# An RWKV scan with two MLPs behind it: operands fetched by another queue, scores loaded in halves, and three steps put in another order

## The reference

```python
for t in range(S):
    y[:, :, t] = np.einsum('bhd,bhde->bhe', rt, state)
    Sa = np.einsum('bhde,bhe->bhd', state, at)
    state_decay = state * wt[:, :, None, :] - np.einsum('bhd,bhe->bhde', Sa, bt)
    state = state_decay + np.einsum('bhd,bhe->bhde', vt, kt)
...
h = x @ w_in                              # 3072 x 320 by 320 x 2048
x = np.maximum(0.01 * h, h) @ w_out       # by 2048 x 320
gate = 1.0 / (1.0 + np.exp(-(x @ w_gate)))
out = (gate * (x @ w_val)) @ w_out2       # 320 x 1536, 1536 x 320
```

## Time and profile before

| | us |
|---|---|
| median of the runs | 1144.23 (1143.53 to 1144.45) |
| profiled execution | 1153.02 |
| its span | 1151.3 |
| PE busy | 1068.9 (93%) |
| DVE busy | 588.7 (51%) |
| ACT busy | 397.3 (35%) |
| POOL busy | 107.2 (9%) |

### The profile page before, as it was taken

How to read it: one execution, slowest core, us unless ns; L and a number is a source line. 1 busy time by engine, 2 the same in 40 slices (tenths; PEclk the granted TensorE clock), 3 DMA queues, 4 the chain that set the end, 5 groups by cost and what they waited for, 6 DMA issues and landing times.

```text
span 1151.3 us, 36471 instructions
## 1 busy us (share of the span) xinstructions
PE 1068.9 (93%) x16102; PEld 913.3 (79%) x16102; DVE 588.7 (51%) x1306; ACT 397.3 (35%) x782; POOL 107.2 (9%) x99
## 2 busy tenths in 40 slices
PE   2477889999999999999999999999999999999998
PEld 1477778888888877777888787888888888888887
DVE  6697957667675765656756123443223232323222
ACT  2232433434444533443342335542223222222222
POOL 6022020202021110101000000000000000000000
PEclk9989879999999999999999999999999999999999
DMA  5648263345436352635243123330100102020000
GB/s 180 207 128 217 60 176 81 115 104 153 122 94 173 91 138 57 166 79 143 43 125 80 42 91 119 106 88 1 60 1 5 55 1 60 1 60 1 23 1 23
DMA packets 134987, 99.82 MB, mean 87 GB/s; under 512 B 96560, under 2 KB 111920, under 8 KB 134832
## 3 DMA queue, kind: packets, MB, share of 16 engines
q1 hardware_dynamic: 132384, 85.06, 27.7%
q0 software_dynamic: 2448, 12.45, 3.1%
HBM read 78.61 MB, written 18.87 MB: 85 GB/s over the span
## 4 chain that ended last, share of the span: by engine, by line
PE 80%; issue 8%; DVE 6%; DMA 2%; POOL 2%; ACT 1%; SPq 1%; ACTq 0%; DVEq 0%; POOLq 0%
PE bank L736 16%; PE bank L787 11%; PE pair L787 11%; PE bank L751 4%; PE bank L807 4%; PE bank L805 4%; PE bank L806 4%; PE bank L752 4%; PE bank L753 4%; DVE prod L1173 2%; DVE t_unit L1177 2%; PE bank L712 2%; PE bank L755 2%; PE bank L756 2%; PE bank L559 2%
## 5 line engine op out<-in xcount | busy, mean ns | idle before, releaser
L1222 DVE TENSOR_TENSOR g_lo<-g_full,g_hi 128x512 fp32r<-128x512 f32 x168 | 120.9, 720 | 243.5 <-ACT g_hi L992 243.4
L992 ACT CAST g_hi<-g_full 128x512 fp32r<-128x512 f32 x168 | 104.4, 621 | 134.7 <-DVE g_full L1274 131.6
L736 PE MATMUL bank<-x_hi,w_up 128*128 128x512 f32 x480 | 136.2, 414 | 2.1 <-issue 2.1
L985 ACT ACTIVATE g_full<-bank 128x512 f32<-128x512 f32 x96 | 57.5, 598 | 215.6 <-PE bank L736 208.7
L1173 DVE TENSOR_TENSOR prod<-t_unit,p_unit 128x126 f32<-128x126 f32 (+22 forms) x372 | 103.6, 278 | 37.3 <-DMA p_unit<-p_dram 26.1
L1177 DVE TENSOR_TENSOR t_unit<-t_unit,prod 128x126 f32<-128x126 f32 (+22 forms) x372 | 105.3, 283 | 12.8
L736 PEld LDWEIGHTS bank<-x_hi,w_up 128*128 128x128 f32 x480 | 86.0, 190 | 21.5 <-issue 2.5
L736 PE MATMUL bank<-x_lo,w_up 128*128 128x512 f32 x288 | 83.7, 400 | 0.0
L1274 DVE TENSOR_TENSOR g_full<-pair,h_sb 128x512 f32<-128x512 f32 x36 | 24.9, 691 | 112.8 <-PE pair L787 112.0
L751 PE MATMUL bank<-g_hi,w_dn 128*128 128x512 f32 x192 | 77.4, 403 | 2.0 <-DVE g_lo L1222 1.8
L752 PE MATMUL bank<-g_hi,w_dn 128*128 128x512 f32 x192 | 75.6, 394 | 0.0
(11 more groups left out here) (143 smaller groups left out, 2357.4 us busy)
## 6 DMA issues: line engine op xcount, KB each, us to landing
b_sb<-in_bF SPq DMA_DIRECT2D x12, 512.0 KB, 6.0
a_sb<-in_aF SPq DMA_DIRECT2D x24, 256.0 KB, 6.4
k_sb<-in_kF SPq DMA_DIRECT2D x12, 512.0 KB, 4.8
p_unit<-p_dram SPq DMA_DIRECT2D x24, 256.0 KB, 4.2
v_sb<-in_vF SPq DMA_DIRECT2D x12, 512.0 KB, 6.7
r_sb<-in_rF SPq DMA_DIRECT2D x12, 512.0 KB, 8.1
w_raw<-in_wF SPq DMA_DIRECT2D x20, 260.0 KB, 3.4
stage<-in_w_out POOLq DMA_DIRECT2D x7, 640.0 KB, 4.5
```

What stands on the lines that cost most here:

```text
L736: last = nc.tensor.matmul(up_bank(m)[:], lhs, rhs, start=(e == 0), stop=(e == len(products) - 1))
L992: nc.scalar.copy(g_hi[:, m % 2], g_full[:]).then_inc(g_hi_ready, 1)
L1222: nc.vector.tensor_tensor(g_lo[:, m % 2], g_full[:], g_hi[:, m % 2].bitcast(F32), ALU.subtract).then_inc(g_lo_ready, 1)
```

## The change

The loads of k, b and a, apart from the first ones, are issued by GpSimd, each just after the wait for the product that frees the buffer (`fetch_k`, `fetch_b`, `fetch_a`, with semaphores of their own); SP keeps the first loads. The scores are read back in two halves of 16 rows, the upper half as soon as they are stored and the columns that used the old upper half are done; the lower half when the inverse before has ended. `inverse_first` waits for the upper half, and column 16 for the lower. `act_t_unit` moves from slot 6 to slot 7, behind the copies of kb. In slot 6 of VectorE `dve_y` comes ahead of `dve_decay`. The first `act_x` moves behind `act_u` of window 2. On SP's queue `store_y(n + 1)` is ahead of `load_w(n + 7)`. Three numbers of `FILL` fall.

```diff
@@ gpsimd_program
+                n = 2 * g
+                if g >= 0:
+                    fetch_k(pool, g + 1)
+                    fetch_b(pool, g + 2)
+                if g == 0:
+                    fetch_a(pool, 4)
+                if unit_in(g + 1):
+                    pool_k(pool, n + 2)
+                if unit_in(g + 2):
+                    pool_b(pool, n + 4)
+                    pool_a(pool, n + 4)
+                if g >= 0:
+                    fetch_a(pool, n + 5)
...
+                if g >= 0:
+                    fetch_a(pool, n + 6)
...
+        def fetch_k(pool, u):
             if unit_in(u):
 
-                multiplied(sp, "kb", 2 * (u - 1) + 1)
-                sp.dma_start(k_sb[:].rearrange("p c q t -> p (c q t)"),
-                             kF[u].rearrange("p c q t -> p (c q t)")).then_inc(k_loaded, 16)
+                multiplied(pool, "kb", 2 * (u - 1) + 1)
+                nc.gpsimd.dma_start(k_sb[:].rearrange("p c q t -> p (c q t)"),
+                                    kF[u].rearrange("p c q t -> p (c q t)")).then_inc(k_fetched, 16)
...
+        def load_p_rows(sp, rows, signal):
+            for z in range(2):
+                sp.dma_start(p_unit[z * MX:(z + 1) * MX, rows].rearrange("p s t -> p (s t)"),
+                             p_dram[:, rows].rearrange("m s t -> m (s t)")).then_inc(signal, 16)
+
+        def load_p_top(sp, u):
             if unit_in(u):
                 sp.wait_ge(p_stored, 128 * (u + 1))
 
+                if u > 0:
+                    sp.wait_ge(column_ready, (C - 1) * (u - 1) + C // 2)
+                load_p_rows(sp, slice(0, C // 2), p_top_loaded)
+
+        def load_p_low(sp, u):
+            if unit_in(u):
+
                 wait(sp, column_ready, (C - 1) * u)
...
@@ FILL
-                ("first", 0): 2, ("cross", 0): 14, ("ut", 0): 4, ("vrur", 0): 6,
+                ("first", 0): 2, ("cross", 0): 2, ("ut", 0): 4, ("vrur", 0): 6,
...
-                ("first", 2): 2, ("cross", 2): 14, ("ut", 2): 4, ("vrur", 2): 4,
+                ("first", 2): 2, ("cross", 2): 4, ("ut", 2): 4, ("vrur", 2): 4,
...
-                ("first", 4): 2, ("cross", 4): 24}
+                ("first", 4): 2, ("cross", 4): 4}
@@ scalar_program
-                    if s == 1 and g % 2 == 0 and 1 <= g // 2 <= NJ:
+                    if s == 1 and g % 2 == 0 and 2 <= g // 2 <= NJ:
                         act_x(act, g // 2 - 1)
...
                             act_u(act, n)
+                            if g == 2:
+                                act_x(act, 0)
                             act_ut(act, n)
...
-                    elif s == 6 and later:
-                        act_t_unit(act, g + 2)
-                    elif s == 7 and soon:
-                        act_kb(act, n + 2)
-                        act_kb(act, n + 3)
+                    elif s == 7:
+                        if soon:
+                            act_kb(act, n + 2)
+                            act_kb(act, n + 3)
+                        if later:
+                            act_t_unit(act, g + 2)
@@ inverse_first, inverse_columns
-            dve.wait_ge(p_loaded, 32 * (u + 1))
+            dve.wait_ge(p_top_loaded, 32 * (u + 1))
...
+                if t == C // 2:
+                    dve.wait_ge(p_low_loaded, 32 * (u + 1))
@@ vector_program, slot 6
-                    elif s == 6 and unit_in(g + 3) and n + 6 >= 4:
-                        dve_decay(dve, n + 6)
...
+                    elif s == 6:
+                        if now:
+                            dve_y(dve, n + 1)
+                        if unit_in(g + 3) and n + 6 >= 4:
+                            dve_decay(dve, n + 6)
```

More of the change, by code:

```diff
@@ L138, in rwkv_mlp_kernel @@
         k_loaded = sem("k_loaded")
+        a_fetched = [sem(f"a_fetched{i}") for i in range(4)]
+        b_fetched = [sem(f"b_fetched{i}") for i in range(2)]
+        k_fetched = sem("k_fetched")
         r_loaded = sem("r_loaded")
@@ L149, in rwkv_mlp_kernel @@
         p_stored = sem("p_stored")
-        p_loaded = sem("p_loaded")
+        p_top_loaded = sem("p_top_loaded")
+        p_low_loaded = sem("p_low_loaded")
         zeros_set = sem("zeros_set")
@@ L286, in pool_a @@
             u, c = divmod(n, 2)
-            pool.wait_ge(a_loaded[n % 4], 16 * (u // 2 + 1))
+            if n < 4:
+                pool.wait_ge(a_loaded[n], 16)
+            else:
+                pool.wait_ge(a_fetched[n % 4], 16 * (n // 4))
             pool.wait_ge(decay_ready, n + 1)
@@ L293, in pool_b @@
             u, c = divmod(n, 2)
-            pool.wait_ge(b_loaded[u % 2], 16 * (u // 2 + 1))
+            if u < 2:
+                pool.wait_ge(b_loaded[u], 16)
+            else:
+                pool.wait_ge(b_fetched[u % 2], 16 * (u // 2))
             pool.wait_ge(inv_ready, n + 1)
@@ L300, in pool_k @@
             u, c = divmod(n, 2)
-            pool.wait_ge(k_loaded, 16 * (u + 1))
+            if u == 0:
+                pool.wait_ge(k_loaded, 16)
+            else:
+                pool.wait_ge(k_fetched, 16 * u)
             pool.wait_ge(inv_ready, n + 1)
@@ L332, in gpsimd_program @@
             for g in range(-2, NU):
[L333 to L338, removed]
+                n = 2 * g
[11 more added lines that the diff above has]
+                    fetch_a(pool, n + 5)
+                if unit_in(g + 1):
+                    pool_k(pool, n + 3)
+                if unit_in(g + 2):
+                    pool_b(pool, n + 5)
+                    pool_a(pool, n + 5)
+                if g >= 0:
+                    fetch_a(pool, n + 6)
                 if g == -1:
-                    pool.wait_ge(p_loaded, 32)
+                    pool.wait_ge(p_low_loaded, 32)
                     for i in range(4):
@@ L408, in store_p @@
                 if c == 0:
-                    wait(sp, p_loaded, 32 * u)
+                    wait(sp, p_top_loaded, 32 * u)
+                    wait(sp, p_low_loaded, 32 * u)
                 dst = p_dram.rearrange("(h i c q) s t -> h i c s q t", h=2, i=2, c=2)
@@ L490, in sync_program @@
             load_a(sp, 1)
-            load_k(sp, 0)
+            load_k(sp)
             load_w(sp, 2)
@@ L498, in sync_program @@
             store_p(sp, 1)
-            load_p(sp, 0)
+            load_p_top(sp, 0)
+            load_p_low(sp, 0)
             load_v_tok(sp, 0)
@@ L1315, in vector_program @@
                         dve_vrur(dve, n + 1)
-                    elif s == 6 and now:
-                        dve_y(dve, n + 1)
+                    elif s == 6:
[3 more added lines that the diff above has]
+                            dve_decay(dve, n + 6)
                     elif s == 7 and later:
```

42 lines of the change are left out of this document (22 added, 20 removed).

## The result

The changed kernel takes 1179.2 us (median of 4 runs, 1176.11 to 1183.31) against 1144.1 us (1143.53 to 1144.45) of the kernel before on the same chip: a ratio of 1.031, 95% interval 1.028 to 1.034, slower by 35 us. The profiled execution took 1179.12 us, its span 1177.1 us.

What follows compares the result with a forecast made beforehand. From 210 us on TensorE's stream of MLP products bounds the kernel; before, engines wait in a ring. Start -16, boundaries +35, clock +15, less 2 absorbed, on the 1144.2 us median gave 1176 us, range 1141 to 1190.

Steps and rivals of the forecast that it cites:

- The start, -16: First three windows, before the MLP has work: first MLP product 16 us earlier, bounds -10 and -21.
- TensorE follows: Window 0: TensorE keeps up with columns starting 7 us earlier, since k is fetched some 7 us earlier.
- the halves of the scores cost nothing at the boundaries: Eight later boundaries: t_unit's store comes some 3 us later, but the zeroing needing it is 9 us later too.
- near 152: Sign of being right: the first MLP product near 152 us.
- its sign of being wrong at this step: Start: first MLP product after 158 us, with GpSimd waiting for k or VectorE for `p_unit`.
- x would bind in window 2: Window 2: x, landing at 158.15, is the next bound; first MLP product at 161.6 instead of 167.66, 6.1 us.
- The link between fills and fetches: Window 0: k is fetched earlier, and the 12 fills removed were 12 of 14 filling TensorE's wait for a, ka.
- The boundaries, +35: Eight boundaries, windows 2 to 9: late zeroing and collisions make TensorE wait for `g_lo`, seven of 4.8 us, one 3.1.
- The four collisions: Each boundary: GpSimd's multiplies k, b, a, k fall on VectorE's columns, 0.92 us each, 3.7 us together.
- rival 3: GpSimd's fetches land 4.3 us later in the first three windows, taking 13 of the 16 back: 1189 us; 8 in 100.
- The clock, +15: Behind the eight boundary waits: clock falls of 2.5 us each, 20, less 5 already there; bounds 0 and +21.
- rival 1: Boundaries: multiplies miss the columns, each costs only the later zeroing's 1.3 us, no clock fall: 1138 us; 17 in 100.

Runs made afterwards that it cites:

- Experiment 8: Experiment 3 with SP's reload of T ahead of the load of the lower half of the scores; 0.997 of the kernel before.
- 10 to 12: Experiment 3 with v, r, v_nu held until k landed and T's reload before the lower half: 0.991; plus decay ahead of y: 0.995; or first x split early: 0.992.
- experiment 12: Experiment 3 with v, r, v_nu held until k landed, T's reload before the lower half, and first x split ahead of the u copies again; 0.992 of the kernel before.
- experiment 3: Changed kernel with t_unit zeroed behind the kb copies only up to g = 1, in slot 6 from window 2 on; 1.000 of the kernel before.
- experiment 4: Changed kernel with GpSimd's multiplies held until column 13 of the inverse from window 2 on, zeroing still late; 1.009 of the kernel before.
- experiment 2: Kernel before with one part of the change alone, the zeroing of t_unit behind the kb copies; 1.039 of the kernel before.
- experiment 9: Kernel before with only the 42 fewer fills of the cross products; 0.997 of the kernel before.
- experiment 1: Changed kernel with the zeroing of t_unit put back in slot 6, ahead of the kb copies, in every window; 1.000 of the kernel before.
- experiment 5: Experiment 3 with SP's loads of v, r and v_nu from window 3 on held until k has landed; 0.993 of the kernel before.

## Why the prediction was right, and where it was off

Forecast 1176 (1141 to 1190), measured 1179.2. The sum was -16 + 35 + 15 - 2 = 32; the profile of the changed kernel gives -9.4 at the start, 30.2 - 1.8 = +28.4 of waits for `g_lo` and 20 - 7 = +13 of clock, together 32 on a profiled execution of 1153.0, which is 1185. The profiled execution was 1179.12, 6 us less. TensorE's idle time from 200 to 800 us apart from the waits for `g_lo` was 14.2 us against 16.7 before, which is 2.5 of the 6, where I had taken 2 off; the rest I can't place, and the clocks, read to 0.01 of twelve windows of 100 us, are no finer than that. That the number came out so near is in part luck: the gain of the start was 6.6 us too large, the waits at the boundaries 6.6 us too large as well, and the two cancel. And the two profiled executions lie only 26.1 us apart, the medians 35.

**The start, -16: mis-sized, 9.4 measured.** Windows 0 and 1 did start their columns earlier: at 49.42 and 94.87, against 57.69 and 105.01, 8.3 and 10.1 us where I had 7 and 9.7. In window 2 they began at 141.19 instead of 149.94. The step that failed is "TensorE follows". It needs not only the scores, but T, and T took longer to come. From the issue of T's store to TensorE's first product with it passed 9.0 and 12.7 us in windows 0 and 1 before, and 11.9 and 15.9 in the changed kernel: at 56.32 TensorE was 0.8 us later than before (55.49), at 102.26 only 2.1 us earlier. SP's timeline of the changed kernel in window 0, and that product:

```profile
84.78 1.09 SPq L459 DMA_DIRECT2D p_unit<-p_dram  x2
86.38 1.25 SPq L482 DMA_DIRECT2D t_dram<-t_unit  x2
87.68 4.26 SPq L459 DMA_DIRECT2D p_unit<-p_dram  x2
93.00 3.52 SPq L493 DMA_DIRECT2D t_sb<-t_dram  x4
...
102.26 0.28 PE L675 MATMUL bank<-rhs_sb,t_sb 32*32 32x40 f32 x2 [3.05 <-issue]
```

T's reload is issued 6.6 us after its store (5.55 before), behind loads of the lower half that took SP 4.26 us to issue, and TensorE starts 9.3 us after that (7.2 before). I had written that the halves of the scores cost nothing at the boundaries, which held, and had not asked what they cost at the start. The order on SP seems to be a part of it: the four profiles with T's reload ahead of the lower half (experiments 8 and 10 to 12) have 10.5 to 11.7 and 13.9 to 15.2 us from store to product, the seven others with SP's new order 11.6 to 15.6 and 15.4 to 16.7, so some 1 to 2 us a window. That still is not the 9.0 and 12.7 of before. In this stretch k and b, 512 KB each, are now in flight beside T; that they are the rest is likely, and no run here shows it. Experiment 8 had the first MLP product at 152.45 us, the "near 152" of the prediction, but 10 to 12, with the same place for T, had 159.34, 163.02 and 156.24. The measured 158.24 is also just beyond the 158 that the prediction had named as its sign of being wrong at this step, though it was T and x_hi that TensorE waited for, and not k or `p_unit`. Also wrong was that x would bind in window 2 as it landed: SP had issued its loads by 142.9 us, and ScalarE's first cast of it began at 155.59, behind the copies of u. By experiment 12 that place is as good as the old one.

The link between fills and fetches was right. Each by itself leaves the first MLP product where it was (167.78 with the fetches and without the fewer fills, 167.82 the other way round); together they bring 10 us in experiment 3 (in the profiles with both, 5 to 15).

**The boundaries, +35: right in mechanism, 28.4 measured.** The 1.3 us of the later zeroing are 1.17 in experiment 4, at seven boundaries. The four collisions are there, and my seven waits of 4.8 us and one of 3.1, 36.7 in all, are 36.1 in experiment 2. In the changed kernel itself the last is 3.13 and four are 4.51 to 5.44, but three only 2.1. The term was too large because I let k land 4.8 us after its issue at every boundary, while at the three with a reload of x it lands late, on the last column (7.9 us in the row read above). My rival 3 priced late fetches as a loss; where the zeroing is late too they shorten the wait, from 5.3 us to 2.1. With the zeroing early the same late fetch is a loss (9.5 us of waits for a in experiment 3).

**The clock, +15: right in sum, +13, by other falls than I had.** I had eight of 2.5 us each. It fell behind the four long waits, for 3.7 to 8.9 us from the product on, half of which is lost, and behind one wait of 2.11 us for x at 721.11. Two windows of the changed kernel, behind the long wait of 328.11 and the short one of 268.44:

```profile
328.00:332.00 4.00, 3.89 (x18) 0.52 0.01 4
...
268.00:272.00 4.00, 3.56 (x96) 1.00 0.02 8
```

Behind the four long waits (4.5 to 5.4 us) the clock stood at its 1.2 GHz level, behind the three of 2.1 us and the one of 3.13 at 2.4 GHz. The length of one wait does not decide it alone: beside that one at 721.11 it fell behind the 2.89 us of experiment 2, and in the kernel before behind a gap of 1.73 us at 432.20. That last one is the 3.3 us at 0.58 which I had put down to the boundary of 425.80.

**What would have changed the sign.** My rival 1 wanted multiplies that miss the columns: experiment 4 has that, and at 1.009 it is still slower, not the 1138 us (0.995) of the rival. The start would have had to bring all 16, and the held multiplies nothing. The Trainium skill, "SBUF — State Buffer" (SBUF: two separate sides), says that VectorE and GpSimd hold their shared port in turns; the 1.13 to 1.73 us of a column beside a multiply of 1.2 agree with it, and experiments 2 and 4 show what it is worth here: 36.1 us of waits against 8.2. The same section's warning, that VectorE can starve the writing of descriptors for DMAs that GpSimd issues, is given there for VectorE operations in a mode that takes both ports, and is borne out by no run here: with v and r held back k landed in 3.6 us from GpSimd's queue.

Four things stay open: which transfers delay T at the start, where the 3.9 us of experiment 9 come from, what the halves of the scores are worth by themselves, which no run tried, and what the reordering of y is worth, which is under what these runs can tell.

## What to carry to other kernels

Before a step is moved behind another on an in-order engine, name for each stage of the program what it waits for and what stands behind it: here the same move took the kb copies out from behind a late DMA at the start, which no median shows as a gain, and put 1.2 us on the critical path at seven boundaries later; an edit by stage (late at the start, early in the dense part) is rid of the second. A delay of 1.2 us that opens room for a collision on a shared port cost 4.6 to 5.1 us of waiting at seven boundaries, 2.9 at the last and, with the clock behind it, 44 us in all (experiment 2). When loads are moved to another queue, look at what they used to stand ahead of: here the order on one queue was also the order of landing, and k lost its place (8.8 us for 5.4).

## What was not expected of the hardware

From the issue of the first store of T (2 issues, 128 KB each) to the reload that waits for it passed 3.6 us in the kernel before and in experiments 2 and 9, and 3.9, 4.0, 5.4, 5.4, 5.4, 5.5, 5.6, 6.1, 6.2, 8.8 and 10.1 us in the changed kernel and the ten made from it. In these the upper half of the scores is loaded right ahead of it and GpSimd fetches k and b beside it; which of the two stretches it was not tried. The next store of T has 5.0 to 5.6 us in the first three kernels and 5.5 to 6.6 in the others, the third 3.6 to 5.1 in both. An in-order wait for a DMA in such a stretch is to be judged by its spread, not by its mean: a 10.1 in one profile can look like the effect of an edit (experiment 1).

Low clock at the start and in the dense part seemed to take turns. Experiment 9 lost 36 us to it before 200 us (0.76, 0.72, 0.80 in windows of 50) and none from 200 to 800; experiment 5 lost 22 (0.88, 0.81, 0.87) and none; the kernel before 19 (0.86, 0.83, 0.93) and 7. With one profile each this is an association and no more. The other profiles without long waits for `g_lo` lost 15 to 27 us before 200 us and 0 to 10 behind it, with no order that holds for all, and the 36 us stand in the run with the lowest clock of experiment 9's twelve.
